# Fewer stops between the long products of a fused attention, dense and expert kernel, and all low parts of w_in made by GpSimd

## The reference

```python
for c in range(nc):                     # chunks of 32 queries
    k_full = concat(mem_k, k[c_start-16 : c_end+8])      # at most 64 keys with the memory's
    scores = scale * q_c @ k_full.T
    a = exp(scores - max); a = a / (sum(a) + 1e-9)
    out[chunk] = a @ v_full
```

## Time and profile before

| | us |
|---|---|
| median of three runs | 832.36 |
| lowest, highest | 832.04, 833.88 |
| the profiled execution, its own time | 831.3 |
| span of its trace | 829.7 |
| PE busy | 817.6 (99%) |
| DVE busy | 508.5 (61%) |
| ACT busy | 467.6 (56%) |
| GpSimd busy | 75.4 (9%) |
| chain that ended last | PE 94%, DVE 2%, issue 1%, ACT 1%, DMA 1% |

### The profile page before, as it was taken

One profiled execution on the slowest core, in us unless ns is written; L12 is line 12 of the kernel. 1 busy time (PEld: TensorE's weight loads), 2 busy tenths in 40 slices (PEclk: granted clock), 3 DMA queues, 4 the chain that ended last, 5 costly groups with the idle time before them and its releaser, 6 DMA issues.

```text
span 829.7 us, 19685 instructions
## 1 busy us (share of the span) xinstructions
PE 817.6 (99%) x8248; PEld 724.1 (87%) x8248; DVE 508.5 (61%) x1021; ACT 467.6 (56%) x824; POOL 75.4 (9%) x96
## 2 busy tenths in 40 slices
PE   7999999999999999999999999999999999999997
PEld 5888888898888888888988898889898999999996
DVE  4678755655565556455655555565644988855563
ACT  3788665655564557655565555565545665544441
POOL 1100000010001001000100010001121342211000
PEclk9999999999999999999999999999999999999999
DMA  7952032204220421322132214202204798556300
GB/s 248 389 138 65 26 116 65 65 27 141 65 65 29 142 73 28 115 66 65 27 115 66 65 27 141 65 2 85 94 13 165 230 376 305 199 209 251 122 15 28
DMA packets 48625, 93.88 MB, mean 113 GB/s; under 512 B 9103, under 2 KB 9103, under 8 KB 48528
## 3 DMA queue, kind: packets, MB, share of 16 engines
q1 hardware_dynamic: 45040, 86.23, 30.9%
q0 software_dynamic: 3488, 6.30, 2.3%
HBM read 78.16 MB, written 17.00 MB: 115 GB/s over the span
## 4 chain that ended last, share of the span: by engine, by line
PE 94%; DVE 2%; issue 1%; ACT 1%; DMA 1%; POOL 0%; POOLq 0%; DVEq 0%; SPq 0%
PE y_ps L916 32%; PE h_ps L902 31%; PE h_ps L1074 10%; PE y_ps L1088 9%; PE s_ps L783 2%; PE s_ps L821 2%; PE turn L844 1%; PE turn L834 1%; PE turn L798 1%; PE s_ps L856 1%; PE turn L943 1%; DMA lists<-pairs,place 1%; PE turn L1029 0%; PE s_ps L1029 0%; DMA xg_b<-x_mid,listed 0%
## 5 line engine op out<-in xcount | busy, mean ns | idle before, releaser
L902 PE MATMUL h_ps<-xT_hi,in_hi 128*128 128x384 f32 x512 | 178.3, 348 | 0.1
L902 PE MATMUL h_ps<-xT_hi,in_lo 128*128 128x384 f32 x512 | 172.3, 337 | 0.0
L902 PE MATMUL h_ps<-xT_lo,in_hi 128*128 128x384 f32 x512 | 171.6, 335 | 0.0
L1167 ACT ACTIVATE us<-h_ps 128x384 f32<-128x384 f32 x128 | 62.4, 487 | 172.2 <-PE h_ps L902 170.3
L916 PE MATMUL y_ps<-out_hi,g_lo 128*128 128x512 f32 x384 | 151.7, 395 | 0.0
L916 PE MATMUL y_ps<-out_lo,g_hi 128*128 128x512 f32 x384 | 151.2, 394 | 0.0
L916 PE MATMUL y_ps<-out_hi,g_hi 128*128 128x512 f32 x384 | 150.7, 392 | 0.4 <-DVE g_lo L1470 0.3
L1464 DVE TENSOR_SCALAR whole<-us 128x384 f32<-128x384 f32 x128 | 47.0, 367 | 109.8 <-ACT us L1167 108.4
L902 PEld LDWEIGHTS h_ps<-xT_hi,in_hi 128*128 128x128 f32 x512 | 96.3, 188 | 3.5 <-DVE xT_lo L1364 0.3
L902 PEld LDWEIGHTS h_ps<-xT_lo,in_hi 128*128 128x128 f32 x512 | 96.4, 188 | 2.3
L902 PEld LDWEIGHTS h_ps<-xT_hi,in_lo 128*128 128x128 f32 x512 | 96.0, 188 | 0.0
(11 more groups left out here) (211 smaller groups left out, 1283.8 us busy)
## 6 DMA issues: line engine op xcount, KB each, us to landing
qk_sb<-qk SPq DMA_DIRECT2D x22, 768.0 KB, 5.2
raw_b<-w SPq DMA_DIRECT2D x32, 512.0 KB, 4.8
raw_a<-w SPq DMA_DIRECT2D x32, 512.0 KB
v_sb<-v SPq DMA_DIRECT2D x22, 512.0 KB, 3.7
x_mid<-x SPq DMA_DIRECT2D x24, 256.0 KB
out<-x SPq DMA_DIRECT2D x24, 256.0 KB
in_raw<-w_in SPq DMA_DIRECT2D x4, 1024.0 KB, 8.0
out_raw<-w_out SPq DMA_DIRECT2D x4, 1024.0 KB, 9.3
```

Of the source, the lines that this page charges most:

```text
L902: last = pe.matmul(h_ps[:, f % 2, 0:BN], w[:, dc, f * P:(f + 1) * P], x[:, half, dc, :], start=(n == 0), stop=(n == 3 * DC - 1))
L1167: act.activation(us[:, f % 2, :], h_ps[:, f % 2, 0:BN], ACT.Copy, scale=1.0 / TWO_PI, bias=0.25).then_inc(us_done, 1)
```

## The change

1. **Tables.** `ATTENTION` is made by a function, `attention(5, 4, 4, 8, 12)`: tile j starts at site 5 + 4j, exp one site later, sum three, probs four, values eight, x twelve. So the tiles overlap in time, and steps of two or three tiles meet at one site. Before, a tile took eight sites and the next began at its end. The router's steps are put at sites 5, 7, 9 to 12, 21 and 22. On PE block 0 then has 6 places instead of 10, each of blocks 1 to 6 has 7 instead of 10, and the last block 4 instead of 7: 52 in all instead of 77. The exps stand at f = 3, 5, 7 instead of 3, 7, 11. sum moves from an odd site (behind `g_low`, with probs) to an even one (f = 4, 6, 8), where DVE does it ahead of `fraction(f)`.
2. **Banks and semaphores.** values and x get halves of s_ps, x1 of j = 1 too, x1T has two buffers, and t_full and t_free become one pair each for probs, x, x1 and ranks. Some new waits come with it: ACT's x step waits for v_free, DVE's first values for s_full, DVE's x1 of j = 1 for s_full.
3. **in_lo.** GpSimd makes all sixteen, and DVE's `in_low` is gone.
4. **Prologue.** The 64 small matmuls are gone, and after the first scores one product of 384 columns stands for two of 512. PE's order ends x 0, x 1, values 2, x 2, with a buffer x_pre of its own for tile 1, instead of x 0, values 2, x 1, x 2. ACT does x 0 and x 1 ahead of its second part of w_in, DVE all sums ahead of its first values. `keep_running(3)` comes after values 2 instead of after x 1.
5. **Loads.** q and k of a tile come by two DMAs instead of one, and q, k and v lie in the host's arrays as one row per partition.
6. **Slots.** `gathered_rows` does three of its four parts ahead of the last ranks instead of two, and `turn_rows(1)` comes at f = 6 instead of 4.

Core of the diff:

```diff
-for _j, _b in enumerate((5, 13, 21)):
-    ATTENTION += [(_b, "scores", _j), (_b + 1, "exp", _j), (_b + 4, "probs", _j), (_b + 4, "sum", _j),
-                  (_b + 6, "values", _j), (_b + 8, "x", _j)]
...
+        b = first + j * period
+        for site, step in ((b, "scores"), (b + 1, "exp"), (b + 3, "sum"), (b + probs, "probs"), (b + values, "values"),
+                           (b + x, "x")):
...
+ATTENTION = attention(5, 4, 4, 8, 12)
...
-            for f in range(AHEAD):
+            for f in range(FT):
                 pool.wait_ge(inhi_done, f + 1)
                 c = slice(f * P, (f + 1) * P)
                 pool.tensor_tensor(in_lo[:, :, c], in_raw[:, :, c], in_hi[:, :, c].bitcast(F32),
-                                   ALU.subtract).then_inc(first_inlo_done, 1)
+                                   ALU.subtract).then_inc(inlo_done, 1)
...
                     if f >= 1 and not has_router(B):
                         out_low(f)
-                        if f + AHEAD < FT:
-                            in_low(f + AHEAD)
...
             pe.wait_ge(ready, 2)
-            for n in range(64):
-                c = slice((n % 4) * 32, (n % 4 + 1) * 32)
-                pe.matmul(turn[c, 0, 0:NL], ident[:, c], ident[:, 0:NL], start=True, stop=True)
...
-                elif (step, j) == ("x", 1):
+                elif (step, j) == ("values", BT - 1):
                     keep_running(turn[:, 0, 0:P], 3)
...
             pe.wait_ge(xg_ld[0], 32)
-            gathered_rows(0)
+            gathered_rows((0, 1, 2))
             pe.wait_ge(route_step, ROUTE * (BLOCKS - 1) + CHOSEN)
             ranks().then_inc(last_ranks_full, 1)
-            gathered_rows(1)
+            gathered_rows((3,))
...
-                    if s == 0 and a == 0 and f == EFT // 2:
+                    if s == 0 and a == 0 and f == EFT - 2:
                         turn_rows(1)
```

More of the change, by code:

```diff
@@ L50 @@
-PROLOGUE_PE = [("scores", 0), ("scores", 1), ("probs", 0), ("scores", 2), ("probs", 1), ("values", 0), ("probs", 2),
[L51 to L55, removed]
@@ L56 @@
-AHEAD = 3
[L57 to L72, removed]
+ORDER = ("values", "x", "probs", "scores", "exp", "sum")
@@ new lines, in attention @@
+def attention(first, period, probs, values, x):
+    sites = {}
+    for j in range(3):
+        b = first + j * period
+        for site, step in ((b, "scores"), (b + 1, "exp"), (b + 3, "sum"), (b + probs, "probs"), (b + values, "values"),
+                           (b + x, "x")):
+            sites.setdefault(site, []).append((step, j))
+    return {site: sorted(steps, key=lambda x: ORDER.index(x[0])) for site, steps in sites.items()}
+ATTENTION = attention(5, 4, 4, 8, 12)
+ROUTER = {5: [("x1", 0), ("x1", 1)], 7: [("logits", 0), ("logits", 1), ("x1", 2)], 9: [("logits", 2)], 10: [("route", 0)],
+          11: [("rexp", 0)], 12: [("gate", 0)], 21: [("ranks", 0)], 22: [("place", 0)]}
@@ new lines @@
+ROUTER_LAST = {5: [("x1", 0), ("x1", 1)], 7: [("logits", 0), ("logits", 1), ("x1", 2)], 9: [("logits", 2)], 10: [("route", 0)],
+               11: [("rexp", 0)], 12: [("gate", 0)], 13: [("ranks", 0)], 14: [("place", 0)]}
+PROLOGUE_PE = [("scores", 0), ("scores", 1), ("probs", 0), ("scores", 2), ("probs", 1), ("values", 0), ("probs", 2),
+               ("values", 1), ("x", 0), ("x", 1), ("values", 2), ("x", 2)]
+PROLOGUE_ACT = [("exp", 0), ("probs", 0), ("exp", 1), ("probs", 1), ("exp", 2), ("probs", 2), ("w_in", 0), ("x", 0),
+                ("x", 1), ("w_in", 1), ("x", 2), ("w_in", 2)]
@@ L75, in program, with steps_of @@
+PROLOGUE_DVE = [("scores", 0), ("scores", 1), ("sum", 0), ("scores", 2), ("sum", 1), ("sum", 2), ("values", 0),
+                ("values", 1), ("x", 0), ("x", 1), ("values", 2), ("x", 2)]
+AHEAD = 3
+def steps_of(B, last):
+    tables = [{} if B == 0 else ROUTER_LAST if B == last else ROUTER,
+              {} if B == last else ATTENTION]
+    return {site: [x for table in tables for x in table.get(site, [])] for site in sorted(set().union(*tables))}
 def program(nc, qk, v, w_in, w_out, w_skip, w_gate, w1, w2, out, x_mid, lists):
@@ L339, in carry, with pieces @@
             eng.sem_inc(carried, 1)
[L341 to L357, removed]
+        def pieces(t):
+            return t.rearrange("p (a c n) -> p a c n", a=2, n=P) if len(t.shape) == 2 else t.rearrange("p a (c n) -> p a c n", n=P)
         last_turn = [turn[:, 0, :], h_ps[:, 0, :], h_ps[:, 1, :]]
@@ L757, in _ @@
         def _(pe):
-            def turn_is_free(B, step, j):
-                wait(pe, t_free, use(B, step, j))
             def attend(B, half, step, j):
```

268 lines of the change are left out of this document (137 added, 131 removed).

## The result

The changed kernel takes 896.77 us, median of four runs (890.65 to 896.99), against 832.2 for the kernel before on the same chip: ratio 1.075, 95% interval 1.0726 to 1.0775. The forecast was 836.0 in a range of 828.0 to 838.0. Its direction was right, its size by far not: +64.6 us instead of +3.7, and outside every case that was priced. The four executions were granted 0.962 to 0.969 of TensorE's full clock, and the trace is from the one that took 896.99.

A forecast was written before the change was run, and what follows sets the result against it. TensorE's work and its stops were taken as the bound (busy 99%). Terms -1.3 + 7.2 - 1.1 - 0.3 - 0.8 = +3.7 took the profiled 831.3 to 835.0, and the median's 1.06 gave 836.0, range 828.0 to 838.0.

The forecast's parts named there:

- I cost them at nothing: Blocks 1 to 6: new waits on v_free and s_full ask for steps two sites or more back, so cost nothing.
- Two DMAs instead of one for q and k cost SP three issues of about 1 us in all at the start: Prologue: the extra issues stand ahead of w_in's issue; part can come back, inside the ends.
- Block 0, the lock: GpSimd's in_lo goes first and excludes VectorE's hs: +0.67 a cycle, 5.4 of the chain's 11.4, plus 0.7 in the first.
- Rival 1: Block 0: GpSimd's subtractions block nothing; block -0.3, sum -3.8, time 828.6; chance 0.24.
- rival 2: Block 0: they exclude each other, but GpSimd only gets VectorE's pauses; block +1.5, time 830.4; chance 0.19.
- Block 0, the tables: Sums 3.6, extra exp 1.9 and extra probs 0.5 join block 0's chain; block 0 in all +7.2.
- Blocks 1 to 6: Fewer exits from places, one more entry, one shape change fewer: -0.19 a block, -1.1 for six.
- Rival 4: Full blocks: merged stops cost the same, so only half the gain comes; 1.1 more, no chance of its own.
- Prologue: First up at 22.8 instead of 24.14: -1.3, ends -0.3 and -2.3.
- Last block and slots: Three places fewer in the last block: -0.3; slots without the 0.82 wait for xg_b: -0.8.
- Rival 3: Blocks 1 to 6: exps make downs late, +3.7; chance 0.07 on rival 1 or 2, 0.03 on the forecast.

The follow-up runs named there:

- fix: The changed kernel with SP issuing q and k of the next tile without waiting behind each load of v: 841.98 us, ratio 1.0111.
- b_poollo: The kernel before with only in_lo changed, all sixteen made by GpSimd: 835.9 us, ratio 1.004.
- best: The kernel of order with block 0's load of the next tile's q and k ahead of w_out's last quarter on SP: 831.32 us, ratio 0.9963.
- best_sum: The kernel of best with the sums back at the odd site beside probs, behind g_low: 830.32 us, ratio 0.995.
- best_pool: The kernel of best with all in_lo on GpSimd: 835.29 us, ratio 1.0008.
- order: The kernel of fix2_dvelo with scores ahead of probs where both meet at one place: 835.55 us, ratio 1.0024.
- b_turn: The kernel before with turn_rows(1) at f = 6 instead of 4 alone: 831.72 us, ratio 0.9983.
- b_latek: The kernel before with q and k of the second tile in blocks 1 to 6 issued only after up(6): 854.88 us, ratio 1.0271.
- fix2_dvelo: The kernel of fix with block 0's late q and k load ahead of SP's small loads and clears, in_lo (f = 3 to 15) on VectorE: 837.45 us, ratio 1.0058.

## Why the prediction was wrong

**The step that failed** is the account of the waits in blocks 1 to 6. It asked only what the new waits of ScalarE and VectorE would cost ("I cost them at nothing"), and of SP's queue it said only "Two DMAs instead of one for q and k cost SP three issues of about 1 us in all at the start". A wait of TensorE for the keys was thus put at nothing without a reason. The new waits did cost nothing: in fix TensorE is busy for 468.95 of the 468.96 us of blocks 1 to 6. But moving the tables also moved what the **old** waits of SP stand for: its loop goes scores, values, scores, values of one tile after the other, and that loop was not walked against the new tables. What was needed was there: a load of q and k took 5.2 to land, by the page of the kernel before,

```profile
qk_sb<-qk SPq DMA_DIRECT2D x22, 768.0 KB, 5.2
```

and a tile's values ended an `up` and a `down` ahead of the next tile's scores, while after the change they stand at the scores' own place. That gives a wait of landing plus issue, about 6, in each block; 5.1 to 6.5 came. Of the 65.6 us between the two spans:

- waits for k_sb: 45.7 (10.8 in block 0, of which 4.3 behind the small loads; 34.9 in blocks 1 to 6)
- the lower pace behind them: in blocks 1 to 6 it is 47.5 - 34.9 - 1.3 (the last is what fix has over before there), 11.3, or 1.9 for each; for the two in block 0 about 4 by the same price, which is an estimate
- the rest, about 4.6: block 0 some 3, which is what its 17.8 leave, blocks 1 to 6 1.3, last block and slots 1.0, prologue -0.8

**Block 0, the lock: mechanism right, size too large.** That GpSimd's subtraction and VectorE's hs exclude each other and GpSimd comes first was shown (b_poollo). In the working it is 8 x 0.67 = 5.4 of the 11.4 in the chain, and the 0.7 of the first cycle, before what is given back; it measured 2.6 and 3.2. Rival 1 (nothing blocks) and rival 2 (GpSimd only gets pauses) are refuted: GpSimd's records stayed at 1.28 and VectorE's grew.

**Block 0, the tables.** Sums, extra exp and extra probs were put at 3.6 + 1.9 + 0.5 = 6.0 of the 11.4. best, with in_lo on VectorE, measured 74.97, +2.4, of which 0.7 is its last wait for keys; 1.3 are the sums (best_sum). Right in kind, too dear for the sums. Both parts together were forecast at +7.2 and measured +5.6 in best_pool.

**Blocks 1 to 6: wrong sign.** The forecast was -0.19 a block, fix measured +0.2. Transposes ahead of small tiles cost 0.17 to 0.23 and not the 0.10 of an entry, three times a block. That explains 0.2 to 0.4 of the 0.4 between forecast and measurement; more closely no run tells. Rival 4, that merged stops cost the same, was nearest. With the other order the places do pay: 77.60 (order) and 77.59 (best) against 77.93.

**Prologue.** -0.8 in the change, and -0.4 to -1.5 in the runs with its prologue, for a forecast of -1.3 with ends of -0.3 and -2.3. The stop of 2.26 for "issue" stayed (2.30). The granted clock differs here from execution to execution: it was 1.00 in the prologue of before and 0.93 in that of the change. The four profiled executions of the new prologue at 1.00 gained 0.9 to 1.5, the five below it 0.4 to 0.9. The 64 small matmuls do not decide that: b_poollo, b_turn and b_latek keep them and had 0.93.

**Last block and slots.** Forecast -0.3 - 0.8 = -1.1 together, measured +1.0 in the change and -0.7 to -1.4 in four other runs. The wait for xg_b was there again at f = 6 in the five kernels that gained nothing. That this came near the forecast in four of them is not a proof of its working, since no edit decides which it is.

**Rival 3** did not come: in fix no `down` of blocks 1 to 6 waits for g_lo.

## What to carry to other kernels

When steps are moved in time, walk every in-order queue through the new order, the load queue above all, even if the diff doesn't touch it: a load that waits behind a wait for something else is late by its whole landing time. A short stall of TensorE costs more than its length, since the clock may fall behind it. Merging stops between long products paid here only when the steps in a stop were put so that small tiles follow small tiles and transposes come last, ahead of the `up` whose tile shape they share.

## What was not expected of the hardware

- Half pace behind waits of only 2.03 to 2.92 us, and not each time: one wait of 2.79, in fix2_dvelo, had none behind it.
- Thirteen subtractions of 128x512 moved from VectorE (0.60 each) to GpSimd (1.28 each) made VectorE busier, not less: 62.00 against 56.46 in block 0.
- On TensorE, going from four transposes to small tiles costs 0.23 (0.59 against 0.36), and from small tiles to transposes about as much, 0.18 (0.79 against 0.66, and 0.41 against 0.36): a stop between long products has a price by its changes of tile shape, not only by being a stop.
- Eight tiny loads and six clears on SP, of about 0.5 each to issue, held back a load that TensorE waited for by 6.9 us (fix: 36.1 to 43.0). Put ahead of them it gained only 1.65 of that, since it then landed 8.9 after its issue instead of 3.9.
